# Queries loaded transposed, with maximum and reciprocal sum of each token spread through DRAM

## The chip, the core and the metric

The kernel runs on one NeuronCore of a Trainium2 chip. Its engines are TensorE (matmuls and transposes, called PE in the profile), VectorE (DVE), ScalarE (ACT), GpSimd (POOL) and SyncE (SP), which here only issues DMA transfers. The metric is the device time of one execution in microseconds.

## The reference

Three layers in a row. With B = 8 batches, H = 8 heads, S = 576 tokens and D = 64 features per head:

```python
q_s = exp(q - max(q, axis=-1));  q_s = q_s / (sum(q_s, axis=-1) + 1e-9)   # over the features
k_s = exp(k - max(k, axis=2));   k_s = k_s / (sum(k_s, axis=2) + 1e-9)    # over the tokens
kv = einsum('bhsd,bhse->bhde', k_s, v)
x  = einsum('bhsd,bhde->bhse', q_s, kv)        # attention output, 4608 x 512 when put together
x  = (relu(x @ w_in) ** 2) @ w_out             # 512 -> 2048 -> 512
x  = rms_norm(x) * rms_g
out = (silu(x @ w_gate) * (x @ w_val)) @ w_out2   # 512 -> 1536 -> 512
```

The softmax of q is over the 64 features of one token, so each token of each head has one maximum and one sum. All is float32.

## The kernel before, in words

**Stages.** The attention of batch 0 runs alone. The first product (x @ w_in) of batch b then runs on TensorE, and the attention of batch b+1 is done between its instructions. When all eight batches are through, `down` (@ w_out), the gated products and the last product follow; the change does not touch these.

**The first product.** A batch's product is cut into PA = 8 groups; a group makes two blocks of 128 outputs for all 576 tokens by a scheme with seven block products instead of eight (names B11, T2, T1, B21, T4, B22, T3). Each block product, `product_a`, is two times three matmuls of 128x128 by 128x288 (lines 1814 to 1816: each number is split in a high and a low part), and is one *step*. A batch has 56 steps. In a group the order is B11, T2, T1, B21, then T4 and B22 of the group before, then T3. After each step TensorE does the attention *rounds* that a table puts there. In batch 0's product, where batch 1's attention is done, all eight products are plain ones (64 steps, `plain`, lines 1835 to 1837).

**The attention in units.** A unit (b, c) is a pair of heads, 128 features; there are KC = 4 per batch, so 28 units beside batch 0. For a unit:
- SyncE loads q (tokens on partitions, 5 tokens and two heads a partition), k with features on partitions (kT), k with tokens on partitions (kt) and v.
- DVE takes the maximum of each token (`qmax`, line 1378), POOL subtracts it (`qsub`, 894), ScalarE takes the exponential (`qexp`, 1082), DVE sums and inverts (`qsum`, `qinv`, 1381 to 1388), POOL multiplies (`qnorm`, 897).
- Round Q0 is three and Q1 two transposes on TensorE (line 1803); ScalarE copies them from the bank to qT (1098). Features are then on partitions.
- Round KM transposes the maxima of k (1791), DVE adds them to kt (1415), ScalarE takes the exponential (1079), round KV multiplies with v and a column of ones (1788, ten instructions), DVE divides and writes a 128x128 block-diagonal matrix bd (1402 to 1410).
- Rounds X0 and X1 multiply bd with the halves of qT (1807); ScalarE copies them to xa (1102), the input of the next batch's product. POOL forms sums of xa (`xa_sums`), ScalarE and DVE split it in high and low parts (`ta_split`).

**What sets the order.** The order on each engine is written out. `UNIT_BASE` gives the step of the previous batch's product that is a unit's zero, and the tables `UNIT_PE`, `UNIT_DVE`, ... give each task's distance from it. Engines wait for one another by semaphores, and each works strictly in its order. DVE also takes the first product's results from the banks: in a group of seven steps `h_u2` comes at place 1, `h_21` (waits for product T4) at place 4, `h_12` (waits for B22) at 5, `h_22` (waits for T3) at 6, each ahead of that step's attention tasks. SyncE has one list for everything, and after each group the two stores of h (`store_h`).

**Banks.** Rounds use two banks of the accumulator in turn (`psR`), so a round waits until the result of the round two before it has been read (`wait_bank`). `taken_by_act` tells who reads which round.

The functions that the diff touches:

Of the kernel before, what the change touches and what calls it, by code (L numbers as in the profile page):

```python
# [12 lines left out]
P = 128  # L13
# [160 lines left out]
def taken_by_act(what):  # L174
    return what not in ("KM", "KV")


def taken_no(n):

    act = taken_by_act(ROUNDS[n][1])  # L180
    return act, sum(taken_by_act(what) == act for _, what, _ in ROUNDS[:n + 1])
# [115 lines left out]
def build(nc, q4_d, q1_d, kT_d, k5_d, v4_d, v1_d, w1_d, s1_d, w2_d, wB_d, gv_d, out):  # L297
    h_d = nc.dram_tensor("h_scratch", [P, CA, B * S], F32, kind="Internal").ap()
    xn_d = nc.dram_tensor("xn_scratch", [P, KC, B * S], F32, kind="Internal").ap()
    a_d = nc.dram_tensor("a_scratch", [P, CB, B * S], F32, kind="Internal").ap()  # L300
    ctx = ExitStack()
    with ctx:
# [81 lines left out]
        vn[1], at = place("vn1", at, [P, SJ, P + 1])  # L384
        assert at <= quad_at
# [5 lines left out]
        qT, at = place("qT", at, [P, S])  # L391
# [4 lines left out]
        qmax, at = place("qmax", at, [P, SJ, 2])  # L396
# [39 lines left out]
        q_sum, q_den, q_inv, q_norm = sem("q_sum"), sem("q_den"), sem("q_inv"), sem("q_norm")  # L436
        rnd_ready, taken_act, taken_dve = sem("rnd_ready"), sem("taken_act"), sem("taken_dve")
# [39 lines left out]
        CONSTS, CONSTS_ALONE, CONSTS_Q = 13, 6, 2  # L477
# [10 lines left out]
        def unit(b, c):  # L488
            return b * KC + c + 1

        def bufs(b, c):

            if b == 0:
                return Bufs(kT_al[:, c], qn_al[:, c], vn_al[:, c], ekS_al[:, c], qT_al[:, c], bd_al[:, c],
                            kmax_al[:, c], qmax_al[:, c])
            i = c % 2
            return Bufs(kT[i][:, :], qn[i][:, :, :, :], vn[i][:, :, :], kt[i][:, :, :], qT[:, :], bd[:, :], kmax[:, :],
                        qmax[:, :, :])

        def loads(b, c):  # L500

            if b == 0:
                return (kT_al_in[c], 16), (q_al_in[c], 32), (v_al_in[c], 32)
            n = (b - 1) * (KC // 2) + c // 2 + 1
            return (kT_in[c % 2], 16 * n), (q_in[c % 2], 32 * n), (v_in[c % 2], 32 * n)

# [113 lines left out]
        def _(sp):  # L620
# [11 lines left out]
            def load_q(b, c):  # L632

                if unit(b, c) > KC + 2:
                    sp.wait_ge(rnd_ready, ROUND_NO[b - (c < 2), "Q1", (c - 2) % KC])
                q = bufs(b, c).q.rearrange("p j h d -> p j (h d)")
                sp.dma_start(q[:, 0:FULL], q4_d[b, c]).then_inc(loads(b, c)[1][0], 16)
                sp.dma_start(q[0:TAIL, FULL], q1_d[b, c]).then_inc(loads(b, c)[1][0], 16)
# [152 lines left out]
            def task(what, b, c):  # L791

                if what in ("q", "kT", "kt", "v"):
                    if unit(b, c) > KC + 2:
                        {"q": load_q, "kT": load_k, "kt": load_kt, "v": load_v}[what](b, c)
                elif what == "s1":
# [67 lines left out]
        def _(pool):  # L864
            done = 0
            for fill in (
# [7 lines left out]
                lambda: nc.gpsimd.memset(qn[0][TAIL:P, FULL], 0.0),  # L874
                lambda: nc.gpsimd.memset(qn[1][TAIL:P, FULL], 0.0),
# [12 lines left out]
            def attention(what, b, c):  # L888
# [180 lines left out]
        def _(act):  # L1069
            def attention(what, b, c):  # L1070
                u = unit(b, c)
                m = bufs(b, c)
                if what == "kexp":
# [10 lines left out]
            def take_round(kind, b, c):  # L1084
# [14 lines left out]
                else:  # L1099
                    if b:  # L1100
                        act.wait_ge(ta_lo, split_a(b - 1, B22))
# [45 lines left out]
            def task(what, b, i):  # L1147

                if what[:4] == "read":
                    if what[4:] not in ("KM", "KV"):  # L1150
                        take_round(what[4:], b, i)
# [212 lines left out]
        def _(dve):  # L1364
            def attention(what, b, c):
# [8 lines left out]
                elif what == "qmax":  # L1374
# [3 lines left out]
                    nc.vector.tensor_reduce(m.qmax, m.q, axis=AX.X, op=ALU.max).then_inc(q_max, 1)  # L1378
# [3 lines left out]
                elif what == "qinv":  # L1382
# [3 lines left out]
                    if u > 1:  # L1386
                        dve.wait_ge(q_norm, u - 1)
                    nc.vector.reciprocal(qinv[:, :, :], qden[:, :, :]).then_inc(q_inv, 1)
# [5 lines left out]
            def take_round(kind, b, c):  # L1394
# [6 lines left out]
                if kind == "KV":  # L1401
# [9 lines left out]
                    last.then_inc(taken_dve, 1)  # L1411
                else:
# [356 lines left out]
        def _(pe):  # L1769
            def do_round(kind, b, c):  # L1770
# [320 lines left out]
```

## Time and profile before

| | us |
|---|---|
| median of 3 runs | 1673.07 (1672.58 to 1673.17) |
| the profiled execution, its own time | 1674.19 |
| its span, first to last instruction | 1672.5 |
| attention of batch 0, alone | to about 31 |
| first product with the attention of batches 1 to 7 | about 31 to 420, some 56 a batch |
| busy in the span: PE / DVE / ACT / POOL | 1651.7 / 1156.5 / 617.1 / 595.0 |

Matmuls are pipelined, so their durations overlap in the records; what one costs the stream is read from start times. Idle time of an engine is given in square brackets in a timeline, with what ended it.

### The profile page before, as it was taken

What the parts mean: (1) busy time and instruction counts of PE and PEld (TensorE: products, weight loads), DVE (VectorE), ACT (ScalarE), POOL (GpSimd) and SP (SyncE); (2) the same over time, 40 slices, a digit from 0 to 9 for tenths busy, and PEclk for the clock granted to TensorE, in tenths of its full rate; (3) what the DMA queues carried; (4) which work ended last, traced back from release to release, by engine and by line L of the source; (5) the groups of instructions that cost most, each with busy time, mean ns of one, the idle gap of its engine ahead of it and who ended that gap; (6) DMA issues with size and microseconds to landing.
All of it is one profiled execution on the core that took longest, in us unless ns stands there. A gap on an engine that the chain in (4) does not pass through costs nothing.

```text
span 1672.5 us, 26402 instructions
## 1 busy us (share of the span) xinstructions
PE 1651.7 (99%) x9926; PEld 1510.2 (90%) x9926; DVE 1156.5 (69%) x1749; ACT 617.1 (37%) x1056; POOL 595.0 (36%) x470
## 2 busy tenths in 40 slices
PE   7999999999999999999999999999999998999999
PEld 6999999999988888888888988988998988999999
DVE  6687667666576778888766565556555568877775
ACT  5544334433333323333334333323333344344432
POOL 3554323332102225342247644556455553000000
PEclk9999999999999999999999999999999999999999
DMA  7685546554553454434342323232331344434441
GB/s 251 195 255 174 173 153 193 173 170 146 201 177 88 121 170 126 119 115 127 113 155 72 104 92 111 91 127 82 107 101 57 104 136 163 140 126 151 150 137 56
DMA packets 151743, 230.07 MB, mean 138 GB/s; under 512 B 11840, under 2 KB 75840, under 8 KB 151616
## 3 DMA queue, kind: packets, MB, share of 16 engines
q1 hardware_dynamic: 151616, 228.38, 42.0%
q8 instruction: 80, 1.31, 0.3%
q14 instruction: 47, 0.39, 0.1%
HBM read 143.39 MB, written 84.93 MB: 137 GB/s over the span
## 4 chain that ended last, share of the span: by engine, by line
PE 92%; DVE 2%; POOL 2%; issue 1%; DMA 1%; ACT 1%; SPq 0%; DVEq 0%; POOLq 0%; ACTq 0%
PE bank L1814 16%; PE bank L1815 16%; PE bank L1816 16%; PE bank L1900 7%; PE bank L1901 7%; PE bank L1902 7%; PE bank L1990 5%; PE bank L1992 5%; PE bank L1991 5%; PE bank L1788 2%; PE bank L1807 2%; PE bank L1803 1%; PE bank L1836 1%; PE bank L1835 1%; PE bank L1837 1%
## 5 line engine op out<-in xcount | busy, mean ns | idle before, releaser
L1814 PE MATMUL bank<-TR,SW 128*128 128x512 f32 (+1 forms) x840 | 308.6, 367 | 0.3 <-DVE TR L1553 0.3
L1816 PE MATMUL bank<-TR,SW 128*128 128x512 f32 (+1 forms) x840 | 308.7, 368 | 0.0
L1815 PE MATMUL bank<-TR,SW 128*128 128x512 f32 (+1 forms) x840 | 308.6, 367 | 0.0
L1814 PE MATMUL bank<-TAR,SA 128*128 128x288 f32 x784 | 248.5, 317 | 0.1
L1815 PE MATMUL bank<-TAR,SA 128*128 128x288 f32 x784 | 231.1, 295 | 0.0
L1816 PE MATMUL bank<-TAR,SA 128*128 128x288 f32 x784 | 230.6, 294 | 0.0
L1900 PE MATMUL bank<-GH,W 128*128 128x512 f32 x576 | 224.2, 389 | 0.4 <-DVE GH L1458 0.4
L1901 PE MATMUL bank<-GH,W 128*128 128x512 f32 x576 | 224.2, 389 | 0.0
L1902 PE MATMUL bank<-GH,W 128*128 128x512 f32 x576 | 224.2, 389 | 0.0
L1145 ACT ACTIVATE GH<-g 128x512 fp32r<-128x512 f32 x144 | 91.1, 633 | 241.6 <-DVE g L1453 159.1
L1990 PE MATMUL bank<-SW,OA 128*128 128x256 f32 x630 | 178.9, 284 | 0.2 <-DVE SW L1627 0.2
L1991 PE MATMUL bank<-SW,OA 128*128 128x256 f32 x630 | 178.8, 284 | 0.0
L1992 PE MATMUL bank<-SW,OA 128*128 128x256 f32 x630 | 178.8, 284 | 0.0
L1814 PEld LDWEIGHTS bank<-TR,SW 128*128 128x128 f32 x840 | 157.7, 188 | 20.6 <-DVE TR L1553 0.6
L1815 PEld LDWEIGHTS bank<-TR,SW 128*128 128x128 f32 x840 | 157.7, 188 | 19.9
L1816 PEld LDWEIGHTS bank<-TR,SW 128*128 128x128 f32 x840 | 157.7, 188 | 19.8
L1458 DVE TENSOR_TENSOR GH<-g,GH 128x512 fp32r<-128x512 f32 x144 | 138.6, 963 | 37.9 <-ACT GH L1145 37.8
L1814 PEld LDWEIGHTS bank<-TAR,SA 128*128 128x128 f32 x784 | 147.2, 188 | 3.4 <-issue 0.4
L1815 PEld LDWEIGHTS bank<-TAR,SA 128*128 128x128 f32 x784 | 147.7, 188 | 2.2
L1816 PEld LDWEIGHTS bank<-TAR,SA 128*128 128x128 f32 x784 | 147.3, 188 | 0.0
L1025 POOL TENSOR_TENSOR group<-group,group 128x512 f32<-128x512 f32 (+1 forms) x60 | 73.1, 1219 | 189.8 <-DVE group L1601 189.4
L1900 PEld LDWEIGHTS bank<-GH,W 128*128 128x128 f32 x576 | 108.1, 188 | 23.3 <-DVE GH L1458 0.8
(176 smaller groups left out, 3340.4 us busy)
## 6 DMA issues: line engine op xcount, KB each, us to landing
h_scratch<-hb SPq DMA_DIRECT2D x128, 288.0 KB, 2.6
hst<-h_scratch SPq DMA_DIRECT2D x144, 256.0 KB, 2.7
araw<-a_scratch SPq DMA_DIRECT2D x18, 1536.0 KB, 6.8
a_scratch<-group SPq DMA_DIRECT2D x72, 256.0 KB, 2.0
xst<-xn_scratch SPq DMA_DIRECT2D x10, 1024.0 KB, 5.4
xn_scratch<-x SPq DMA_DIRECT2D x9, 1024.0 KB, 5.4
a_scratch<-group SPq DMA_DIRECT2D x48, 192.0 KB, 1.9
out<-ost SPq DMA_DIRECT2D x36, 256.0 KB, 2.0
```

The costliest lines, as they stand in the source:

```text
L1025: nc.gpsimd.tensor_tensor(a1, a1, val1, ALU.mult).then_inc(a1_done, 1)
L1145: nc.scalar.activation(GH[:, r % GH_RING, 0], g[:, r % G_RING], ACT.Copy).then_inc(ghi_done, 1)
L1458: nc.vector.tensor_tensor(GH[:, r % GH_RING, 1], g[:, r % G_RING], f(GH[:, r % GH_RING, 0]), ALU.subtract)\
L1814: nc.tensor.matmul(ps[:, 0:w], w_hi[:, cc], x_hi[:, c], start=opens and c == 0, stop=False, skip_group_check=True)
L1815: nc.tensor.matmul(ps[:, 0:w], w_lo[:, cc], x_hi[:, c], start=False, stop=False, skip_group_check=True)
L1816: last = nc.tensor.matmul(ps[:, 0:w], w_hi[:, cc], x_lo[:, c], start=False, stop=c == 1, skip_group_check=True)
L1900: nc.tensor.matmul(acc[c][:, :], W2[:, j, 0, cc], GH[:, r % GH_RING, 0], start=j == 0, stop=False, skip_group_check=True)
L1901: nc.tensor.matmul(acc[c][:, :], W2[:, j, 1, cc], GH[:, r % GH_RING, 0], start=False, stop=False, skip_group_check=True)
L1902: last = nc.tensor.matmul(acc[c][:, :], W2[:, j, 0, cc], GH[:, r % GH_RING, 1], start=False, stop=j == CA - 1, skip_group_check=True)
L1990: nc.tensor.matmul(ps, a_hi, w_hi, start=start, stop=False, skip_group_check=True)
L1991: nc.tensor.matmul(ps, a_lo, w_hi, start=False, stop=False, skip_group_check=True)
L1992: last = nc.tensor.matmul(ps, a_hi, w_lo, start=False, stop=stop, skip_group_check=True)
```

## The change

For the units of batches 1 to 7:
- The queries are loaded a second time with features on partitions (`load_qT`, one transfer of 128x576). The load with tokens on partitions is laid out anew: partition p holds tokens 5p to 5p+4 of both heads (115 partitions, and the last token on a 116th); it serves only for maximum and sum.
- `qmax` and `qinv` are written side by side into qs (two buffers). SyncE stores them in DRAM (`store_qs`, 116 partitions of 4 rows of 5 numbers) and loads them back with one row repeated on the 64 partitions of a head: `load_max` into qmax_all and `load_inv` into qinv_all, two transfers each. Both buffers are single, so load_max waits for the unit before's `qTsub` and load_inv for the read of its X1.
- POOL subtracts the maxima from qT (`qTsub`), ScalarE takes the exponential (`qTexp`). POOL's `qnorm`, rounds Q0 and Q1 and ScalarE's copies of them are gone.
- DVE, not ScalarE, reads X0 and X1, and multiplies by the reciprocal sums in doing so.
- Places in the tables: the unit bases become 13, 23, 33, 44 for batch 1 (were 10, 22, 33, 44) and 11, 18, 28, 39 for the others (were 8, 17, 28, 39); the loads and the work on q with tokens on partitions are earlier by 3, relative to the base.

```diff
-UNIT_BASE = [[10, 22, 33, 44]] + [[8, 17, 28, 39]] * (B - 2)
-UNIT_PE = [("KM", -3), ("Q0", 0), ("Q1", 1), ("KV", 2), ("X0", 6), ("X1", 7)]
-UNIT_DVE = [("qmax", -10), ("qsum", -6), ("qinv", -6), ("kmax", -9), ("readKM", -2), ("readKV", 3)]
-UNIT_ACT = [("qexp", -7), ("kexp", -1), ("readQ0", 1), ("readQ1", 2), ("readX0", 7), ("readX1", 8)]
-UNIT_POOL = [("qsub", -9), ("qnorm", -4)]
-UNIT_SP = [("q", -20), ("kT", -19), ("kt", -17), ("v", -15)]
+SHARE = S // SJ
+UNIT_BASE = [[13, 23, 33, 44]] + [[11, 18, 28, 39]] * (B - 2)
+UNIT_PE = [("KM", -3), ("KV", 2), ("X0", 6), ("X1", 7)]
+UNIT_DVE = [("qmax", -13), ("qsum", -9), ("qinv", -9), ("kmax", -9), ("readKM", -2), ("readKV", 3), ("readX0", 7), ("readX1", 8)]
+UNIT_ACT = [("qexp", -10), ("kexp", -1), ("qTexp", 3)]
+UNIT_POOL = [("qsub", -12), ("qTsub", 1)]
+UNIT_SP = [("q", -23), ("kT", -19), ("kt", -17), ("v", -15), ("qT", -9), ("store_qs", -7), ("load_max", -3), ("load_inv", 2)]
...
-def taken_by_act(what):
-    return what not in ("KM", "KV")
+def taken_by_act(b, what):
+    return what not in (("KM", "KV", "X0", "X1") if b else ("KV",))
...
+                    if later(b, c) > 2:
+                        sp.wait_ge(q_sum, unit(b, c) - 2)
+                    else:
+                        sp.wait_ge(const_done, CONSTS_Q1)
+                    q = bufs(b, c).q.rearrange("p j h d -> p (j h) d")
+                    sp.dma_start(q[0:SHARE], q5_d[b - 1, c]).then_inc(loads(b, c)[1][0], 16)
+                    sp.dma_start(q[SHARE:SHARE + 1, 0:2 * SJ:SJ], qe_d[b - 1, c]).then_inc(loads(b, c)[1][0], 16)
+            def load_qT(b, c):
+                if later(b, c) > 2:
+                    sp.wait_ge(rnd_ready, ROUND_NO[b - (c < 2), "X1", (c - 2) % KC])
+                sp.dma_start(bufs(b, c).qT, qT_d[b - 1, c]).then_inc(qT_in[c % 2], 16)
+            def store_qs(b, c):
+                sp.wait_ge(q_inv, unit(b, c))
+                rows = qs_d[unit(b, c) - 1].rearrange("k (p j) -> p k j", j=SJ)
+                sp.dma_start(rows[0:SHARE + 1], qs[0:SHARE + 1, c % 2, :, :]).then_inc(qs_st[c % 2], 16)
+            def spread(b, c, to, first, done):
+                for h in range(2):
+                    row = qs_d[unit(b, c) - 1, first + h:first + h + 1, 0:S]
+                    sp.dma_start(to[h * D:(h + 1) * D, :], row.to_broadcast([D, S])).then_inc(done, 16)
+            def load_max(b, c):
+                sp.wait_ge(qs_st[c % 2], 16 * ((later(b, c) + 1) // 2))
+                if later(b, c) > 1:
+                    sp.wait_ge(qT_sub, later(b, c) - 1)
+                spread(b, c, qmax_all, 0, max_in)
+            def load_inv(b, c):
+                if later(b, c) > 1:
+                    sp.wait_ge(taken_dve, taken_no(ROUND_NO[b - (c < 1), "X1", (c - 1) % KC] - 1)[1])
+                spread(b, c, qinv_all, 2, inv_in)
...
+                elif what == "qTsub":
+                    pool.wait_ge(qT_in[c % 2], 16 * ((b - 1) * (KC // 2) + c // 2 + 1))
+                    pool.wait_ge(max_in, 32 * later(b, c))
+                    nc.gpsimd.tensor_tensor(bufs(b, c).qT, bufs(b, c).qT, qmax_all[:, :], ALU.subtract).then_inc(qT_sub, 1)
...
+                elif what == "qTexp":
+                    act.wait_ge(qT_sub, later(b, c))
+                    nc.scalar.activation(m.qT, m.qT, ACT.Exp).then_inc(qT_exp, 1)
...
+                elif kind in ("X0", "X1"):
+                    cols = slice(int(kind[1]) * TA, (int(kind[1]) + 1) * TA)
+                    dve.wait_ge(ta_lo, split_a(b - 1, B22))
+                    dve.wait_ge(inv_in, 32 * later(b, c))
+                    nc.vector.tensor_tensor(xa[:, c, cols], ps[:, 0:TA], qinv_all[:, cols], ALU.mult).then_inc(taken_dve, 1)
...
                     wait_taken(pe, ROUND_NO[b, "KV", c] - 1)
-                    wait_taken(pe, ROUND_NO[b, "Q1" if half else "Q0", c] - 1)
+                    if b:
+                        pe.wait_ge(qT_exp, later(b, c))
+                    else:
+                        wait_taken(pe, ROUND_NO[b, "Q1" if half else "Q0", c] - 1)
                     last = nc.tensor.matmul(ps[:, 0:TA], m.bd, m.qT[:, half * TA:(half + 1) * TA], start=True, stop=True)
```

`later(b, c)` counts the units from batch 1 on, from 1. The order of the rounds in a batch's 56 steps becomes: 8 KM0; 13 KV0; 15 KM1; 17 X0 of u0; 18 X1 of u0; 20 KV1; 24 X0 of u1; 25 X1 of u1, KM2; 30 KV2; 34, 35 X of u2; 36 KM3; 41 KV3; 45, 46 X of u3.

## Rows read from the trace of the kernel before

**Rows 1.** The page, part 1: busy us (share), instructions.
```profile
PE 1651.7 (99%) x9926; PEld 1510.2 (90%) x9926; DVE 1156.5 (69%) x1749; ACT 617.1 (37%) x1056; POOL 595.0 (36%) x470
```
**Rows 2.** Windows: stretch: length, busy by engine (instructions), PEclk, DMA share, GB/s.
```profile
32.00:40.00 8.00, 7.16 (x55) 6.96 (x54) 5.54 (x10) 4.00 (x8) 2.52 (x2) 1.00 0.89 298
...
208.00:264.00 56.00, 56.00 (x419) 54.90 (x419) 38.74 (x89) 21.52 (x48) 18.98 (x13) 1.00 0.52 170
```
**Rows 3.** The chain of waits in order of time: start, us, what.
```profile
211.56 0.33 PE bank L1803 x3
213.69 1.34 PE bank L1788 x10
...
223.82 1.12 PE bank L1788 x10
...
267.40 0.33 PE bank L1803 x3
```
**Rows 4.** Timeline of TensorE around a unit: start, us, instruction.
```profile
221.12 0.29 PE L1814 MATMUL bank<-TAR,SA 128*128 128x288 f32 x1
...
221.52 0.49 PE L1803 MATMUL bank<-ident,qn 128*128 128x128 f32 x3
...
222.24 0.30 PE L1814 MATMUL bank<-TAR,SA 128*128 128x288 f32 x1
...
222.64 0.38 PE L1803 MATMUL bank<-ident,qn 128*128 128x128 f32 x2
...
223.26 0.30 PE L1814 MATMUL bank<-TAR,SA 128*128 128x288 f32 x1
...
230.12 0.29 PE L1814 MATMUL bank<-TAR,SA 128*128 128x288 f32 x1
...
231.02 0.30 PE L1814 MATMUL bank<-TAR,SA 128*128 128x288 f32 x1
```
**Rows 5.** Line 1803: durations min/median/max; and the timeline at its first later round.
```profile
L1803 PE MATMUL bank<-ident,qn x140: 270/271/329, 39.9 to 413.3; 128*128 128x128 f32 x140
...
38.81 0.29 PE L1837 MATMUL bank<-TAR,SA 128*128 128x288 f32 x1
39.95 0.52 PE L1803 MATMUL bank<-ident,qn 128*128 128x128 f32 x3 [0.84 <-POOL qn L897]
```
**Rows 6.** Groups by line and form, 0 to 560 us: busy us, mean ns, idle before.
```profile
L1504 DVE TENSOR_TENSOR hb<-hb,bank 128x288 f32<-128x288 f32 x56 | 25.4, 454 | 1.9
...
L914 POOL TENSOR_TENSOR xa<-xa 128x576 f32<-128x576 f32 x7 | 10.1, 1436 | 0.0
...
L1128 ACT ACTIVATE TAR<-xa 128x576 fp32r<-128x576 f32 x46 | 30.3, 676 | 12.9 <-POOL xa L920 12.9
```
**Rows 7.** Timelines of TensorE and DVE: end of T4, h_21; then an X round.
```profile
202.33 0.29 PE L1816 MATMUL bank<-TAR,SA 128*128 128x288 f32 x1
...
202.66 0.46 DVE L1491 TENSOR_TENSOR hb<-hb,bank 128x288 f32<-128x288 f32 x1 [0.61 <-PE bank L1816]
203.03 0.93 DVE L1438 TENSOR_TENSOR TAR<-xa,TAR 128x576 fp32r<-128x576 f32 x1
...
227.57 0.29 PE L1814 MATMUL bank<-TAR,SA 128*128 128x288 f32 x1
...
228.85 0.29 PE L1814 MATMUL bank<-TAR,SA 128*128 128x288 f32 x1
```
**Rows 8.** Timelines of SyncE's queue and DVE where the first unit's store would go.
```profile
31.86 2.85 SPq L652 DMA_DIRECT2D SA<-in_w  x5
...
38.24 0.22 DVE L1388 RECIPROCAL qinv<-qden 128x10 f32<-128x10 f32 x1
```
**Rows 9.** DMA issues: count, KB each, median us from issue to landing.
```profile
h_scratch<-hb SPq DMA_DIRECT2D x128, 288.0 KB, 2.6
...
kT<-in_kT SPq DMA_DIRECT2D x28, 288.0 KB, 3.7
...
gv<-in_gv SPq DMA_DIRECT2D x1, 2.0 KB, 6.2
```

More of the change, by code:

```diff
@@ L171 @@
 N_ALONE = len(ALONE_PE) - 1
-def taken_by_act(what):
-    return what not in ("KM", "KV")
+def taken_by_act(b, what):
+    return what not in (("KM", "KV", "X0", "X1") if b else ("KV",))
 def taken_no(n):
-    act = taken_by_act(ROUNDS[n][1])
-    return act, sum(taken_by_act(what) == act for _, what, _ in ROUNDS[:n + 1])
+    act = taken_by_act(*ROUNDS[n][:2])
+    return act, sum(taken_by_act(b, what) == act for b, what, _ in ROUNDS[:n + 1])
 NR = NT * CA
@@ L384, in build @@
         vn[1], at = place("vn1", at, [P, SJ, P + 1])
+        qT = [None] * 2
+        for i in range(2):
+            qT[i], at = place(f"qT{i}", at, [P, S])
         assert at <= quad_at
@@ L390, in build @@
             kt[i], at = place(f"kt{i}", at, [P, SJ, P])
-        qT, at = place("qT", at, [P, S])
+        qmax_all, at = place("qmax_all", at, [P, S])
+        qinv_all, at = place("qinv_all", at, [P, S])
         bd, at = place("bd", at, [P, P])
@@ L505, in loads, with later @@
             return (kT_in[c % 2], 16 * n), (q_in[c % 2], 32 * n), (v_in[c % 2], 32 * n)
+        def later(b, c):
+            return unit(b, c) - KC
         def round_bank(n):
@@ L632, in load_q @@
             def load_q(b, c):
[L634 to L638, printed above, removed]
+                if b == 0:
+                    q = bufs(b, c).q.rearrange("p j h d -> p j (h d)")
+                    sp.dma_start(q[:, 0:FULL], q4_d[c]).then_inc(loads(b, c)[1][0], 16)
+                    sp.dma_start(q[0:TAIL, FULL], q1_d[c]).then_inc(loads(b, c)[1][0], 16)
+                else:
[6 more added lines that the diff above has]
+                    sp.dma_start(q[SHARE:SHARE + 1, 0:2 * SJ:SJ], qe_d[b - 1, c]).then_inc(loads(b, c)[1][0], 16)
@@ L795, in task @@
                         {"q": load_q, "kT": load_k, "kt": load_kt, "v": load_v}[what](b, c)
+                elif what == "qT":
+                    load_qT(b, c)
+                elif what == "store_qs":
+                    store_qs(b, c)
+                elif what == "load_max":
+                    load_max(b, c)
+                elif what == "load_inv":
+                    load_inv(b, c)
                 elif what == "s1":
@@ L1149, in task @@
                 if what[:4] == "read":
-                    if what[4:] not in ("KM", "KV"):
+                    if taken_by_act(b, what[4:]):
                         take_round(what[4:], b, i)
@@ L1377, in attention @@
                         dve.wait_ge(q_sub, u - 1)
-                    nc.vector.tensor_reduce(m.qmax, m.q, axis=AX.X, op=ALU.max).then_inc(q_max, 1)
+                    if b and later(b, c) > 2:
+                        dve.wait_ge(qs_st[c % 2], 16 * ((later(b, c) - 1) // 2))
+                    nc.vector.tensor_reduce(m.qmax.rearrange("p j h -> p (j h)"), m.q.rearrange("p j h d -> p (j h) d"),
+                                            axis=AX.X, op=ALU.max).then_inc(q_max, 1)
                 elif what == "qsum":
@@ L1385, in attention @@
                     dve.wait_ge(q_den, u)
-                    if u > 1:
-                        dve.wait_ge(q_norm, u - 1)
-                    nc.vector.reciprocal(qinv[:, :, :], qden[:, :, :]).then_inc(q_inv, 1)
+                    if b == 0:
+                        if u > 1:
+                            dve.wait_ge(q_norm, u - 1)
+                        nc.vector.reciprocal(qinv[:, :, :], qden[:, :, :]).then_inc(q_inv, 1)
+                    else:
+                        if later(b, c) > 2:
+                            dve.wait_ge(qs_st[c % 2], 16 * ((later(b, c) - 1) // 2))
+                        nc.vector.reciprocal(qs[:, c % 2, 2:4, :].rearrange("p k j -> p (k j)"),
+                                             qden[:, :, :].rearrange("p j h -> p (j h)")).then_inc(q_inv, 1)
                 else:
@@ L2069 @@
     k1 = np.concatenate([k1, k4[:, :, TAIL:, FULL - 1]], axis=2)
+    heads = q.reshape(B, KC, 2, S, D)[1:]
     arrays = {
-        "q4": q4,
-        "q1": q1,
+        "q4": q4[0],
+        "q1": q1[0],
+        "q5": np.ascontiguousarray(heads[:, :, :, 0:SHARE * SJ].reshape(B - 1, KC, 2, SHARE, SJ, D).transpose(0, 1, 3, 2, 4, 5))
+        .reshape(B - 1, KC, SHARE, 2 * SJ, D),
+        "qe": np.ascontiguousarray(heads[:, :, :, SHARE * SJ:].transpose(0, 1, 3, 2, 4)),
+        "qT": np.ascontiguousarray(heads.transpose(0, 1, 2, 4, 3)).reshape(B - 1, KC, P, S),
         "kT": np.ascontiguousarray(k.reshape(B, KC, 2, S, D).transpose(0, 1, 2, 4, 3)).reshape(B, KC, P, S),
```

20 lines of the change are left out of this document (11 added, 9 removed).

## The prediction

> **What bounds the kernel now.** I began with the page's busy shares: TensorE is busy 99% of the span [rows 1]. That row counts overlapping matmuls, so I went on to the stretch table: in 56 us of the attention-and-first-layer stage TensorE has no idle time, DVE is busy 38.7 us, POOL 19.0, and the DMA engines half the time; the granted clock is full, 2.4 GHz [rows 2]. The chain of waits settles it: it runs through TensorE's own instructions, batch after batch, and the same transposes come back after 267.40 - 211.56 = 55.84 us [rows 3]. So each batch's period is the sum of what TensorE streams; an instruction taken from it shortens the period unless a wait comes in its place. Third I read TensorE's timeline by start times, since durations overlap there [rows 4].
>
> **Notation.** One step is one product_a (six matmuls). A batch has 56 steps. u0 to u3 are the four attention units (pairs of heads) of the next batch, worked in between. E13 is the moment at which TensorE has streamed the product of step 13.
>
> **Part 1: five transposes less per unit.** Q0 and Q1 go. Half a product, three matmuls, takes 0.40 us (221.12 to 221.52). Q0 begins at 221.52, and the next product's second half at 222.24: 222.24 - 221.52 - 0.40 = 0.32 us for three transposes and the slower matmul behind them. Q1: 223.26 - 222.64 - 0.40 = 0.22 us [rows 4]. That is 0.54 us a unit, 28 units: -15.1 us. One wait goes too: in the first unit of a batch the KV round takes 1.34 us on the chain instead of 1.12 [rows 3]; its bank is that of Q0, which ScalarE has to read first, and now the round two before it is long read. -0.22 x 6 batches = -1.3. And TensorE's 0.84 us wait for POOL's normalization in the first unit of all goes [rows 5].
>
> A row and a page differ here. The profile gives each transpose a duration of 271 ns [rows 5], but five of them move the stream by 0.54 us only. The Trainium skill, "TensorE: Matmul & The Clock Gate", Part 4, gives about 275 ns for a 128x128 transpose in a kernel's context. By that the 140 transposes would be worth some 38 us; it is a rival below.
>
> **Part 2: X is read by DVE, with the factor.** A DVE operation on a bank of 128x288 takes 454 ns [rows 6], so eight reads add 3.6 us of DVE to 38.7 in a period of 54: no bound. ScalarE loses its copies and gets one exp of 128x576, about 676 ns; POOL's normalization becomes a subtraction of 128x576, 1436 ns [rows 6], about what it was. None of these is on the chain.
>
> But the order of DVE's work is written out, and a bank is now given back later. The banks of the rounds are two, so a round waits for the read of the round two before it. In the new order step 24 ends with X0 of u1, step 25 with X1 of u1 and, right behind it, KM of u2 (28 - 3). KM of u2 takes the bank of X0 of u1. DVE reads that at its step 25, which is the fifth of a group of seven, where h_21 comes first, and h_21 waits for the T4 product that TensorE does in this same step 25. From rows: take s as the start of T4's last matmul (202.33). DVE starts h_21 at s+0.33 and its next operation 0.37 later (203.03), so the read of X0 would run s+0.70 to s+1.15. TensorE streams T4 to s+0.13, X1 costs 227.57 to 228.85 less two halves of products, 1.28 - 0.80 = 0.48, so it is at KM at s+0.61 [rows 7]. It waits 0.54 us, and refilling its pipe costs about one weight load more: I take 0.7 us, once in each of 6 batches: +4.2. Bounds: 0 if the read slips in front of h_21, 1.2 if KM's weights and the next product refill in full. In the batch done beside the plain stage the same pair (step 30) has DVE waiting for the product of step 29, not 30, and fits. KM of u3 comes two steps after X0 of u2, which is enough (2.1 us against 1.6).
>
> **Part 3: the way through DRAM.** Per unit SyncE issues six more transfers: qT, one store of 116 x 20 numbers, four spreading loads. At 0.57 us each [rows 8] that is 14 us more in a period of 54, which alone delays nothing. The cost is in when they land. The trace has no load of one DRAM row into 64 partitions; the nearest, kT with the same 2304 bytes a partition, lands in 3.7 us, a store of h in 2.6, and the smallest, gv (16 bytes a partition) in 6.2 [rows 9]. So 2.6 to 6.2; I take 3.7 for a pair, counted from the second issue.
>
> The tightest unit is u1, whose base lies only 7 steps behind u0's. SyncE has k's load for u2 (step 11) in its queue, and that waits for the KV round of u0, which moved from step 10 to 13. So SyncE stands until E13+1.3 (KV costs 1.12 [rows 3], and its last matmul's tail). Behind it are that load (0.5), load_inv of u0 (1.1), v of u2 in two parts (1.2), two h stores (0.8), and load_max of u1, whose second issue starts at E13+5.5 and lands at E13+9.2. POOL's subtraction and the exp [rows 6] bring it to E13+11.4. TensorE reaches X0 of u1 after 11 steps and KV, KM, X0, X1, KV, with KM's cost 231.02 - 230.12 - 0.80 = 0.10 [rows 4]: 8.8 + 1.12 + 0.10 + 0.96 + 1.12 = 12.1. Slack 0.7 us. load_inv of u0 (second issue E13+2.3) lands at E13+6.0; DVE reads it at E13+6.3, and TensorE would feel that only 1 us later. load_inv of u1 waits for DVE's read of X1 of u0 and lands about 1.5 us before its use. Nobody is late, but with little to spare; the other units have 4 us or more. SyncE's h stores go out some 4 us later, with two groups of buffers behind them. I take 0 for all this, with an upper bound of (6.2 - 3.7 - 0.7) = 1.8 us a batch, 10.8 in all.
>
> The first unit has no slack. Its reciprocal is ready at 38.46 as before, but five weight loads issued from 31.86 on [rows 8] (2.62 MB, at 298 GB/s and 89% of the DMA engines [rows 2] until about 41), and qT, are ahead of its store, so this lands at about 43. load_max's second issue at 43.6 plus 2.6 to 3.7 gives 46.8; subtraction and exp until 48.9. TensorE ends step 10's product at 38.94 (38.81 plus 0.13, [rows 5]) and is at X0, after step 19, at 38.94 + 0.10 + 4.0 + 1.12 + 3.2 = 47.4. Wait about 1.4 us (0 to 4). SyncE is held meanwhile, and s1's load and sums come later: 0.4 more.
>
> **Sum.** Batches 2 to 7: 6 x (-2.16 - 0.22 + 0.70) = -10.1. Batch 1: -2.16 - 0.84 + 1.4 + 0.4 = -1.2. Together -11.3 us. The profiled execution took 1674.19 us (span 1672.5), 1.1 more than the median of 1673.07; 1674.19 - 11.3 - 1.1 = 1661.8 us. What follows the stage is the same work, earlier.
>
> **Rivals.**
> - No new bank wait: DVE's read fits before TensorE gets to KM. For: DVE idles half the time. Against: h_21 is ahead of it in a fixed order. 1661.8 - 4.2, and with a milder start, 1657.
> - Some waits of the spread data: 3.7 us is a median, and the DMA share of 52% [rows 2] comes in bursts. 0.7 to 1.2 us a batch more: 1666 to 1669.
> - Slower than before: the round trip through DRAM is the wait that takes the transposes' place, at X0 of u1 in every batch. It decides once a spreading pair needs over 3.7 + 0.7 = 4.4 us; beyond that each microsecond is one on the chain in each of 6 batches, and before's time is met at 6.3. With 7.5 us it gives 1661.8 + 6 x 3.1 = 1680. For: 64 reads of one row, 464 pieces of 20 bytes, and gv's 6.2 us. Against: kT and h, thirty times the store's bytes and twice a spreading load's, land in 3.7 and 2.6.
> - DVE becomes the bound where it is fullest, beside the plain stage and at batch ends, and eats the gain: about 1672. Against it: it has 17 us idle per period, and kmax leaves the dense end of the batch (step 55 becomes 2 of the next).
> - Transposes are worth their durations: 28 x 5 x 0.271 = 38 us, 1636. The start times speak against it.
>
> The Trainium skill, "DMA: Bandwidth & Descriptors", "Why a DMA increments its semaphore by 16 and not by 1", says that a transfer runs on the largest number of engines up to 16 that divides its outermost dimensions; 116 rows would then use 4 engines, and q's 115 rows 5. All transfers of before have multiples of 16, so no row here shows it. It would put the load of q and the store on few engines; it speaks for the slower rival, though q has ten steps to land.
>
> **Chances.** Forecast 0.56 (its own range 1658 to 1666); no new wait 0.16; some waits 0.13; slower 0.10; DVE 0.04; durations 0.01. 80% range: 1656 (nothing in the transposes' place: 15.1 + 1.3 + 0.8 = 17.2) to 1671. A measurement of this kernel tells 0.2%, 3.3 us, from no change. Faster by more: 0.56 + 0.16 + 0.01 + 0.07 of the waits = 0.80; within: 0.09; slower: 0.11.
>
> **What would show it.** Period of a batch from transposed maxima to the same: 54.1 to 54.3 us instead of 55.84. TensorE idle before KM (the transpose of kmax) about 0.5 to 0.7 us once a batch, released by DVE's read of a bank; none before X0, save once near 47 us, released by ScalarE's exp of qT. SyncE's queue: spreading loads landing in 3 to 4.5 us. Wrong if X rounds wait for the exp in each batch, if DVE waits long for the spread reciprocals, or if the period shrinks by under 1 us.

## The result, and the profile after

Median 1765.95 us of 4 runs (1761.81 to 1775.03), beside 1672.97 for the kernel before: ratio 1.0563, 95% interval 1.0544 to 1.0581. The change costs 93 us; 1661.8 was predicted. The profiled execution took 1768.66 us, span 1766.9.

The page, parts 1 and 4 [rows 1]. TensorE has 140 instructions less and DVE is no busier in share, but the chain that ended last now runs for 10% of the span through transfers (1% before), most of it the store of qs and the spread of the reciprocals:

```profile
PE 1675.7 (95%) x9786; PEld 1523.8 (86%) x9786; DVE 1186.2 (67%) x1805; ACT 593.8 (34%) x972; POOL 598.6 (34%) x470
...
PE 75%; DMA 10%; DVE 6%; POOL 3%; SPq 2%; issue 2%; ACT 1%; DVEq 0%; POOLq 0%; ACTq 0%
PE bank L1893 12%; PE bank L1895 12%; PE bank L1894 12%; PE bank L1979 7%; PE bank L1980 7%; PE bank L1981 7%; PE bank L2069 5%; PE bank L2070 5%; PE bank L2071 5%; DMA qs_scratch<-qs 4%; DMA qinv_all<-qs_scratch 3%; DVE TAR L1514 2%; DMA qmax_all<-qs_scratch 1%; PE bank L1864 1%; PE bank L1886 1%
```

Windows, columns as in [rows 2]. The stretch 208 to 264 has no idle TensorE before; now it loses 6.6 us. At 48 to 64 TensorE stands, and with it so idle the granted clock falls to 0.63 and 0.52 of 2.4 GHz; in the second stretch it is nearly all the time at the lower level, 1.2 GHz:

```profile
48.00:56.00 8.00, 3.70 (x10) 2.61 (x10) 0.00 (x0) 1.39 (x3) 1.40 (x1) 0.63 0.78 254
56.00:64.00 8.00, 4.90 (x22) 4.90 (x23) 4.12 (x7) 3.10 (x4) 4.07 (x5) 0.52 0.74 144
208.00:264.00 56.00, 49.41 (x350) 47.37 (x350) 39.62 (x87) 15.53 (x30) 16.42 (x11) 0.98 0.75 210
```

The period of a batch, read from the starts of the first unit's transposed maxima (line 1867), is 78.2 us for the first and then 64.6 to 74.4; before it is 59.8 and then 55.8 to 56.8. The first product ends at 572.5 us instead of 476.8, so all of the loss lies ahead of that. From 27 us to there, TensorE is idle for 74.4 us (1.7 before), and the granted clock is at 1.2 GHz for 78.5 us, in 16 falls, with TensorE busy in 66.1 of them (never before). At that level ten matmuls of a KV round take 2.16 us instead of 1.12, so I estimate this at half of 66.1, 33 us. Idle time and clock are thus 106 us more, and the stage is 96 us longer: what is left, 10 us, is gained.

DMA issues, median us to landing [rows 9]. Not only are the new transfers slower than the 3.7 I took; the old ones are too (h was 2.6, kT 3.7):

```profile
h_scratch<-hb SPq DMA_DIRECT2D x128, 288.0 KB, 5.0
...
kT<-in_kT SPq DMA_DIRECT2D x28, 288.0 KB, 6.1
...
qmax_all<-qs_scratch SPq DMA_DIRECT2D x56, 144.0 KB, 4.1
qinv_all<-qs_scratch SPq DMA_DIRECT2D x56, 144.0 KB, 5.0
```

Waits between 40 and 420 us (who waited for whom: us, times, longest). The round trip ends at TensorE in two places: at the X round (line 1886) by way of the exp, and, since DVE's read of X (1487) waits for the spread reciprocals, at the next rounds that need its bank, KV (1864) and the transpose of kmax (1867). The product (1893) waits for DVE's split. PE and PEld rows of one line show one wait twice; one of them is shown:

```profile
POOL qT L955 <- DMA qmax_all<-qs_scratch: 139.4, 21, 9.6
...
DVE xa L1487 <- DMA qinv_all<-qs_scratch: 33.3, 10, 10.8
...
PE bank L1886 <- ACT qT L1143: 21.4, 11, 4.7
PEld bank L1893 <- DVE TAR L1514: 21.1, 11, 6.8
...
PEld bank L1867 <- DVE xa L1487: 13.5, 6, 4.3
...
PEld bank L1864 <- DVE xa L1487: 11.8, 5, 2.9
```

The chain in the first unit, and then in a later batch: the store of 9 KB takes 7.55 us to land, the spread of the reciprocals 7.44. SyncE stands for the store, and everything behind it is late. It is no start-up effect: counted from the semaphore events of the trace, the 28 stores land in 3.8 to 10.3 us, 7.5 in the median:

```profile
37.55 7.55 DMA qs_scratch<-qs
45.12 0.46 SPq L674
...
51.03 7.44 DMA qinv_all<-qs_scratch
58.59 0.47 DVE xa L1487
...
197.74 2.16 PE bank L1864 x10
...
200.79 6.92 DMA qinv_all<-qs_scratch
...
212.01 8.72 DMA qs_scratch<-qs
...
225.12 6.94 DMA qs_scratch<-qs
```

And one row that I took long to read rightly, from the timeline of SyncE's queue (start, length of the issue). The issue right behind the store of qs (line 668) takes 6.59 us, where issues take about 0.5:

```profile
143.72 0.34 SPq L668 DMA_DIRECT2D qs_scratch<-qs  x1
144.12 6.59 SPq L641 DMA_DIRECT2D kt<-in_k  x1
150.75 0.59 SPq L694 DMA_DIRECT2D vn<-in_v  x1
```

### The profile page after: what moved, and what is told of

Read it like the earlier page. It is cut to its first block, busy times and chain, and to the rows that moved or that the text cites. A ratio compares the mean times of both kernels' runs of the same rounds, so it can differ in the third digit from the quotient of the medians.

```text
span 1766.9 us, 26259 instructions
## 1 busy us (share of the span) xinstructions
PE 1675.7 (95%) x9786; PEld 1523.8 (86%) x9786; DVE 1186.2 (67%) x1805; ACT 593.8 (34%) x972; POOL 598.6 (34%) x470
## 3 DMA queue, kind: packets, MB, share of 16 engines
q8 instruction: 78, 1.28, 0.3%
## 4 chain that ended last, share of the span: by engine, by line
PE 75%; DMA 10%; DVE 6%; POOL 3%; SPq 2%; issue 2%; ACT 1%; DVEq 0%; POOLq 0%; ACTq 0%
PE bank L1893 12%; PE bank L1895 12%; PE bank L1894 12%; PE bank L1979 7%; PE bank L1980 7%; PE bank L1981 7%; PE bank L2069 5%; PE bank L2070 5%; PE bank L2071 5%; DMA qs_scratch<-qs 4%; DMA qinv_all<-qs_scratch 3%; DVE TAR L1514 2%; DMA qmax_all<-qs_scratch 1%; PE bank L1864 1%; PE bank L1886 1%
## 5 line engine op out<-in xcount | busy, mean ns | idle before, releaser
L1893 PE MATMUL bank<-TAR,SA 128*128 128x288 f32 x784 | 254.1, 324 | 21.9 <-DVE TAR L1514 16.8
L1894 PE MATMUL bank<-TAR,SA 128*128 128x288 f32 x784 | 237.8, 303 | 0.0
L1895 PE MATMUL bank<-TAR,SA 128*128 128x288 f32 x784 | 237.1, 302 | 0.0
L1893 PEld LDWEIGHTS bank<-TAR,SA 128*128 128x128 f32 x784 | 154.2, 197 | 27.9 <-DVE TAR L1514 25.0
L1894 PEld LDWEIGHTS bank<-TAR,SA 128*128 128x128 f32 x784 | 154.2, 197 | 2.7
L1895 PEld LDWEIGHTS bank<-TAR,SA 128*128 128x128 f32 x784 | 153.6, 196 | 0.0
```

The lines of the kernel that those rows point to most:

```text
L1893: nc.tensor.matmul(ps[:, 0:w], w_hi[:, cc], x_hi[:, c], start=opens and c == 0, stop=False, skip_group_check=True)
L1894: nc.tensor.matmul(ps[:, 0:w], w_lo[:, cc], x_hi[:, c], start=False, stop=False, skip_group_check=True)
L1895: last = nc.tensor.matmul(ps[:, 0:w], w_hi[:, cc], x_lo[:, c], start=False, stop=c == 1, skip_group_check=True)
```

## Experiments

Each was timed in 3 rounds against the kernel before, which stayed at 1672.6 to 1673.2. Intervals are of the ratio to it.

**Is it the layout on 115 and 116 partitions?** Edits to the changed kernel; x128 is both, b_q115 puts q's layout alone into the kernel before (the tokens then stand in another order, and the output isn't the reference's; the same holds for b_tr, b_trW and b_trn below).

```diff
# q128 (q5 padded with zeros past row 116)
-sp.dma_start(q[0:SHARE], q5_d[b - 1, c]).then_inc(loads(b, c)[1][0], 16)
-sp.dma_start(q[SHARE:SHARE + 1, 0:2 * SJ:SJ], qe_d[b - 1, c]).then_inc(loads(b, c)[1][0], 16)
+sp.dma_start(q, q5_d[b - 1, c]).then_inc(loads(b, c)[1][0], 16)
# s128
-sp.dma_start(rows[0:SHARE + 1], qs[0:SHARE + 1, c % 2, :, :]).then_inc(qs_st[c % 2], 16)
+sp.dma_start(rows, qs[:, c % 2, :, :]).then_inc(qs_st[c % 2], 16)
```

> The changed kernel (1766 us), with the token-major q of later batches as one load of 128 partitions x 2560 bytes (rows past the 116th are zeros) instead of 115 partitions and a small rest. Theory F (few engines: a transfer whose partition count is no multiple of 16 moves through few DMA engines and holds up everything queued behind it there): most of the 93 us goes, 1680 to 1715, transfers land in 3 to 5 us instead of 5 to 7. Theory V (volume: 25 MB more are too much for the stage): no change, 1760 to 1772. Theory L (the round trip through DRAM has too little slack whatever the queues do): 1745 to 1766.

> The changed kernel, with only the store of maxima and reciprocals done from 128 partitions instead of 116. Theory F with the blame on the store's 464 small pieces: 1690 to 1730. If the q load is what clogs, the store itself saves at most 1 us a unit: 1745 to 1766. Theories V and L: 1760 to 1770.

> Both of the above together. Theory F: 1662 to 1700, at its best the 1662 that was predicted. Theory V: 1760 or so. Theory L: 1740 to 1765.

> The kernel before, with nothing changed but the q load of later batches: 115 partitions x 2560 bytes and a rest, as in the changed kernel (its tokens are permuted for it, the rest of the computation is left as it was). Theory F: transfers behind the q loads land later (4 to 7 us instead of 2.6 to 3.7), but the loads have slack, so 1673 to 1690. Theories V and L: 1673, landing times unchanged.

Measured: q128 1723.34 us (1.0276 to 1.0311), s128 1729.88 (1.0317 to 1.0352), x128 1712.34 (1.0218 to 1.0248), b_q115 1672.84 (0.999 to 1.0009). So the layout is 53.6 us of the 93. Either half brings most of it (42.6 and 36.1), and q's layout costs nothing in a queue that has room. What is left in x128 is 39 us. Theory F had more in mind: q128 and x128 end above its ranges, s128 just inside; b_q115 separates none of the theories.

**Places in the tables, on x128.** x128_split puts DVE's split of B22 first in its step. x128_sp moves two loads later. x128_all is both, with X0 read a step earlier; x128_allb also moves batch 1's units to 16, 26, 35, 45.

```diff
# x128_split
-table.setdefault(start_of(b) + n - STEPS, []).append((what, b, i))
+tasks = table.setdefault(start_of(b) + n - STEPS, [])
+tasks.insert(0 if table is DVE_AT and i == B22 else len(tasks), (what, b, i))
# x128_sp
-UNIT_SP = [("q", -23), ("kT", -19), ("kt", -17), ("v", -15), ...
+UNIT_SP = [("q", -23), ("kT", -19), ("kt", -12), ("v", -11), ...
```

> The x128 kernel (1712 us), with DVE's B22 split ahead of that step's sum, reciprocal and maximum of u1 and the maxima of k, instead of behind them. Theory O (order: what is left of the loss is tasks on DVE and SyncE standing behind another unit's wait): the wait of TensorE for DVE's TAR (33 us in all in x128) goes for the most part; 12 to 18 us less, 1695 to 1702. Theory D (DMA traffic as such, landings of 4 to 6 us, sets the time): 1708 to 1713, since the waits for spread data take the place.

> The x128 kernel, with kt and v loaded 5 and 4 steps later than now (kt -12, v -11), so that SyncE no longer stands before load_max of u1 until the KV round of u0 is through. Theory O: TensorE's wait at X0 of u1, 2.9 us a batch in the trace, goes, but the wait for the B22 split stays: 1695 to 1706. Theory D: 1708 to 1713, since the spreading loads then land just as late beside others.

> Both orders mended, and DVE's read of X0 one step earlier (readX0 at 6), ahead of h_21, so that KM of u2 finds its bank free. Theory O: 6 batches at about 54.3 to 55 us a period instead of 60.6; what stays is the start of batch 1, some 10 us: 1668 to 1680. Theory D: 1700 to 1712.

> As x128_all, with the units of batch 1 placed 3 steps later (2 the third, 1 the fourth), for the first store that lands late behind the weight loads. Theory O: 3 to 6 us less than x128_all, 1664 to 1675. If the start's delay comes in by SyncE's queue and its late s1 loads and not by the unit's own chain: within 1 us of x128_all.

Measured: 1703.83 (1.017 to 1.020), 1728.26 (1.0321 to 1.0351), 1728.80 (1.031 to 1.0358), 1726.09 (1.0299 to 1.0345). The split gains 8.5 us, less than the 12 to 18 I expected: the 33 us of that expectation add the rows of weight load and matmul, which are one wait, 19.9 us between 30 and 480 us. The later loads lose 16, against my expectation, and x128_all and x128_allb, which contain them, end some 50 us above theirs. A reason stands in the waits of SyncE's queue for the store's landing between 100 and 420 us, x128 first, then x128_sp: it now reaches load_max early and stands there with the other loads behind it. That this is the whole of the 16 us is not shown.

```profile
SPq L673 <- DMA qs_scratch<-qs: 29.0, 12, 4.0
```
```profile
SPq L673 <- DMA qs_scratch<-qs: 59.5, 16, 6.1
```

The chain of x128 (start, us, what) shows three ways in which the rest is lost: the split (1513) behind maxima and sums of u1 (1441, 1445), for which TensorE is idle 2.05 us; the round trip, which X0 (1885) waits for, 0.20 us here and 1.64 in the batch before; and the transpose of kmax (1866) behind DVE's read of X0, 0.43 us. A fourth is not on this chain: at 252.56 the KV round is idle for 1.75 us until DVE has read a bank of X (1486).

```profile
234.13 0.74 DVE qs L1441
234.94 1.27 POOL qn L950
...
237.01 0.83 DVE qden L1445
...
238.82 0.76 DVE TAR L1513
...
248.68 6.22 DMA qmax_all<-qs_scratch
255.04 1.45 POOL qT L954
256.51 0.70 ACT qT L1142
...
257.34 0.72 PE bank L1885 x2
...
259.26 0.46 DVE xa L1486
259.77 0.32 PE bank L1866
```

**More lead for the round trip.** On x128_split: maxima, sums and store four steps earlier, in the first unit 11; load_max 2 to 8 steps earlier. DVE's read of X0 also moves one step earlier, and kt and v are loaded 3 and 2 steps later. d_best also has batch 1's units at 16, 26, 35, 45.

```diff
# d_lead; LEAD holds the places of the first two units of batches 2 to 7
+LEAD = {"q": {0: -34}, "qmax": {0: -24}, "qsub": {0: -23}, "qexp": {0: -21}, "qsum": {0: -20}, "qinv": {0: -20},
+        "store_qs": {0: -18}, "load_max": {0: -11, 1: -5}}
-UNIT_DVE = [("qmax", -13), ("qsum", -9), ("qinv", -9), ...
+UNIT_DVE = [("qmax", -17), ("qsum", -13), ("qinv", -13), ...
+UNIT_SP = [("q", -27), ("kT", -19), ("kt", -14), ("v", -13), ("qT", -9), ("store_qs", -11), ("load_max", -6), ("load_inv", 2)]
```

> x128 (both few-partition transfers mended) with DVE's B22 split first in its step, and the chain of the maxima and sums (qmax, qsub, qexp, qsum, qinv) and the store of qs placed 4 steps earlier, for the first unit of a batch 11; load_max 3 to 8 steps earlier, and load k 3 later, v 2 later. Theory O (order and slack: what is left is the round trip that comes due before its data, and DVE's in-order work behind the maxima): the 31 us between 1703.8 and 1673 go for the most part, 1670 to 1690. Theory V (the added traffic itself fills the queue; lead does not help): it stays at 1700 or above.

> d_lead with batch 1's units at steps 16, 26, 35, 45 instead of 13, 23, 33, 44, so that the first round trip has three steps more. Theory O: batch 1 loses some 10 us at 40 to 64 us in x128; 3 to 8 us below d_lead. Theory V: like d_lead, within 3 us.

Measured: 1695.74 (1.0123 to 1.016) and 1690.88 (1.0089 to 1.015). Together these moves help by 8 us, 13 with batch 1's places (the two intervals overlap). d_lead ends above its 1670 to 1690, d_best 4.9 us below d_lead as expected, and 18 us above the kernel before: slack alone isn't all.

**The traffic without its use.** The kernel before with every transfer of the change, and nobody who uses what they bring. The units keep the places of the kernel before, and the store and load_max come 3 steps later, relative to the unit, than in the change. b_tr doesn't wait for the store and spreads rows of the input; in b_trW SyncE waits, and the rows come from the scratch in DRAM, as in the change. b_tr128 is b_tr with q as before and the store from 128 partitions; b_trn is b_tr without the spreading loads.

```diff
# b_tr: store of constants, spreading loads from the input
+sp.dma_start(qTx[:, :], qT_d[b - 1, c]).then_inc(qTx_in, 16)
+sp.dma_start(rows[0:SHARE + 1], src[0:SHARE + 1]).then_inc(qs_st[c % 2], 16)
+for h in range(2):
+    sp.dma_start(to[h * D:(h + 1) * D, :], row.to_broadcast([D, S])).then_inc(done, 16)
# b_trW, ahead of the loads of the maxima
+sp.wait_ge(qs_st[c % 2], 16 * ((n + 1) // 2))
```

> The kernel before with all transfers of the change added to it, at the change's places relative to the unit: q in 115 and 1 partitions (its tokens are permuted, so the output is not the reference's), qT, a store of 116 x 20 numbers (constants) per unit and four spreading loads. No engine uses what they bring, and SyncE never stands for the store's landing. Theory V (traffic alone): most of the 93 us, 1730 to 1765. Theory D (the wait for the round trip and who stands behind it): 1673 to 1685, landings of the other loads 1 to 2 us longer and hidden, as with the q load alone.

> As b_tr, but SyncE waits for the store's landing before it loads the spread maxima back, as in the change; nothing else waits for these transfers. Theory D in the form that SyncE's standing still holds up the other loads behind it: 1690 to 1730. In the form that only the users of the spread data wait (POOL, then TensorE at X0): within 10 us of b_tr. Theory V: the same as b_tr.

> b_tr with q in its old layout of 128 partitions and the store from 128 partitions; the same volume within 2%, no user, no wait for the store. Theory F (transfers of 115 and 116 partitions clog the queue, SyncE's issues then stand 5 to 8 us, and the h stores behind them come late): no issue over 3 us and 1673 to 1685. Theory V (volume): 1710 or above, with landings as in b_tr (6 to 8 us).

> b_tr without the four spreading loads per unit; q in 115 and 1 partitions, qT and the store of 116 partitions stay. If the layout of q and the store is enough to clog the queue: still 1710 or above, with issues of 5 us. If it needs the spreading loads as well (q's layout alone cost nothing in b_q115): 1673 to 1690.

Measured: b_tr 1731.39 (1.0335 to 1.0366), b_trW 1758.42 (1.0482 to 1.0523), b_tr128 1680.04 (1.003 to 1.0067), b_trn 1683.8 (1.005 to 1.0086). This settles the largest part. Traffic that nobody waits for costs 58 us; SyncE's standing for the store, with the rows from the scratch, 27 more (above all its ranges); and with 128 partitions the same traffic costs 7.4. The volume is nearly free, the layout isn't, and it needs a full queue: without the spreading loads it costs 11.

Timeline of SyncE's queue, b_tr and then b_tr128. The load of v stands for 5.51 us behind the 116-partition store, and not behind the other:

```profile
203.13 0.27 SPq L665 DMA_DIRECT2D qs_scratch<-ident  x1
203.45 5.51 SPq L684 DMA_DIRECT2D vn<-in_v  x1
```
```profile
220.28 0.38 SPq L658 DMA_DIRECT2D qs_scratch<-ident  x1
220.71 0.58 SPq L677 DMA_DIRECT2D vn<-in_v  x1
```

Counted in these timelines between 40 and 470 us, issues directly behind the store against all others: b_tr 21 of 27 over 2 us, mean 4.14, others 0.51; the changed kernel 11 of 24, mean 2.94, others 0.52; q128 10 of 27, mean 1.68; with the store on 128 partitions (s128, x128, b_tr128, d_best) none of 27 each, mean 0.55 to 0.64. The table of waits puts some of this down to TensorE, since v's load also names its semaphore; but the KV round that it needs had ended 3.8 to 13.5 us before the issue began in every one of the long ones, and in the changed kernel, where k's load is the one behind the store, 1.5 to 8.8 us. What suffers is in b_tr's waits: h's buffers come free late, so ScalarE reads the product banks late, and batch 0's sums get their data late.

```profile
ACT hb L1211 <- DMA h_scratch<-hb: 53.1, 12, 8.9
...
POOL SA L967 <- DMA SA<-in_s: 35.2, 7, 8.4
```

Windows of b_tr and of b_tr128: the DMA share is 0.82 and 0.89, they move 208 and 226 GB/s, and TensorE loses 4.1 and 1.4 us. The mended layout moves more in the same time, not less.

```profile
208.00:264.00 56.00, 51.88 (x388) 50.44 (x386) 35.47 (x82) 20.03 (x44) 17.68 (x12) 1.00 0.82 208
```
```profile
208.00:264.00 56.00, 54.58 (x407) 53.24 (x407) 37.07 (x85) 20.62 (x46) 17.44 (x13) 1.00 0.89 226
```

**One spread instead of two.** e_one, on d_best: the logarithm of the sums is added to the maxima, one number per token is spread, X needs no factor.

```diff
+nc.scalar.activation(qden[:, :, :], qden[:, :, :], ACT.Ln).then_inc(q_ln, 1)
+nc.vector.tensor_tensor(qm, qm, qden[:, :, :].rearrange("p j h -> p (j h)"), ALU.add).then_inc(q_inv, 1)
-spread(b, c, qinv_all, 2, inv_in)
```

> d_best with two spreading loads per unit instead of four: ScalarE takes the logarithm of the sums, DVE adds it to the maxima, that sum is stored (2 rows of numbers instead of 4) and spread, and exp(qT - spread) is the normalized query. X needs no factor and is read by ScalarE as in the kernel before. Theory V2 (what is left of the loss in d_best, 18 us, is queue volume and the load on DVE): 1672 to 1683. Theory O (it is the round trip itself, its latency): within 4 us of d_best, 1687 to 1695.

Measured 1692.2 (1.0097 to 1.0129), as d_best. The second spread's waits are gone, but the logarithm has its own price: ScalarE's timeline has 61 table loads of 1.28 us (ACT_TABLE_LOAD), 28 of them ahead of the logarithms and most others ahead of the exponentials that follow, where d_best has 5. The chain has 1.10 us of one on ScalarE just ahead of the logarithm of 0.21 and, behind both, the read of a product bank for which TensorE waits:

```profile
224.31 1.10 ACT L1148
225.61 0.21 ACT qden L1148
225.82 0.31 ACT hb L1242
226.17 0.40 PE bank L1897
```

**Finer places, and a queue of its own.** f_fine, on d_best: u0's maximum and sum 5 steps earlier, u1 one step later with its sum behind the split, reciprocals loaded as soon as the buffer is free. g_act is d_best with store and spreads issued by ScalarE; h_act is g_act with f_fine's places in batches 2 to 7.

```diff
# f_fine
-UNIT_BASE = [[16, 26, 35, 45]] + [[11, 18, 28, 39]] * (B - 2)
+UNIT_BASE = [[16, 26, 35, 45]] + [[11, 19, 28, 39]] * (B - 2)
+        "load_inv": {0: -5, 1: 1, 2: 0, 3: -2}, "readX0": {0: 7}}
# g_act
-sp.dma_start(to[h * D:(h + 1) * D, :], row.to_broadcast([D, S])).then_inc(done, 16)
+nc.scalar.dma_start(to[h * D:(h + 1) * D, :], row.to_broadcast([D, S])).then_inc(done, 16)
```

> d_best, and: maximum and sum of the first unit of a batch 5 steps earlier (out of the splits at the end of the batch before), those of the second unit behind the split of B22, the second unit one step later (its X0 and the next KM then take different banks one step apart), and the loads of the reciprocals issued as soon as the buffer is free (in the first unit 7 steps earlier). Theory O (the rest is DVE's order and the second spread's latency): a batch takes 54 to 55 us instead of 56.1, batch 1 loses 3 us less: 1675 to 1682. Theory V (queue volume): within 4 us of 1690.9.

> d_best with the store of qs and the four spreading loads issued by ScalarE on a queue of its own, at the same steps; SyncE keeps all other transfers. If the shared queue holds the round trip up (it lands in 4 to 5 us behind other loads, and SyncE stands for the store while loads wait behind it): the store and the spreads land in 2.5 to 3.5 us and the time falls to 1670 to 1682. If the DMA engines themselves are the limit: landings stay at 4 to 5 us, 1687 to 1695. Should ScalarE's standing for the store hold up its reads of the product banks: above 1695.

> g_act with f_fine's places for batches 2 to 7 (maximum and sum of the first unit earlier, the second unit one step later, reciprocals loaded as soon as their buffer is free). Shared queue as the cause: 2 to 8 us below g_act, as the wait for the reciprocals of the second unit goes. Engines as the cause: within 3 us of g_act. ScalarE standing: as g_act or worse.

Measured: 1693.2 (1.0107 to 1.0167), 1715.79 (1.0231 to 1.0266), 1727.96 (1.0309 to 1.034). f_fine fails: the waits only change places. g_act answers the question of the queue. On ScalarE's own queue the two spreads together land no sooner than in d_best (4.0 and 4.9), so it isn't SyncE's queue alone that holds them:

```profile
qmax_all<-qs_scratch ACTq DMA_DIRECT2D x56, 144.0 KB, 4.8
qinv_all<-qs_scratch ACTq DMA_DIRECT2D x56, 144.0 KB, 4.2
```

ScalarE's standing for the store comes on top: TensorE's product waits 14.3 us in 12 waits for ScalarE's reads of the banks between 40 and 480 us (5.1 in 7 in d_best). That this is all of the 25 us over d_best is not shown. In h_act the X rounds wait 30.2 us in 6 waits behind DVE's work on kt, a loss of its own. No version beat the kernel before.

## Why the prediction was wrong

**Part 1, the transposes: right.** 0.54 us a unit. Chain of the kernel before, KV of u2 and of u3, then of d_best where nothing waits: 11.50 and 10.96 us for the same 11 steps.

```profile
235.31 1.12 PE bank L1788 x10
246.81 1.12 PE bank L1788 x10
```
```profile
248.58 1.12 PE bank L1868 x10
259.54 1.12 PE bank L1868 x10
```

Over 28 units that is an estimate of 15 us, and in every version it is eaten; the count over the stage of the changed kernel leaves 10. The 271 ns of a transpose in the records, and the Trainium skill's about 275 ("TensorE: Matmul & The Clock Gate", Part 4), are not what one costs the stream.

**Part 2, DVE: place right, bounds too small.** DVE takes 452 ns for an X, as taken. KM waits for DVE's read of X0, forecast at 0.7 us a batch, 4.2 in all: 13.5 us in 6 waits in the changed kernel, since X0 itself is late there; in x128 it is still 10.1 in 8. The KV round, which needs such a bank too, I had not priced: 11.8 us in 5 waits. And I left out DVE's written order: when maxima are late, the split of B22 stands behind them (21.1 us of waits; in x128 16.8, and 8.5 us back with the order changed). "No bound" was argued from DVE's busy share, and that says nothing of an engine that works in order.

**Part 3, the round trip: this step failed.** I wrote "I take 0 for all this", with 1.8 us a batch as upper bound, and of the six more transfers a unit that the time to issue them "alone delays nothing". All three signs that I had named for being wrong came: X rounds wait for the exp, DVE waits for the reciprocals up to 10.8 us, and the period grows. Three terms were wrong.
- The landing of the new transfers was taken from rows of a half-empty queue. DMA share was 0.52 [rows 2]; the traffic of the change takes it to 0.75, and a spread lands in 4.1 to 5.0 where I took 3.7. The maxima's 4.1 would still have fitted the 4.4 us that I named as the turning point, and the reciprocals' 5.0 is about what the 1 to 1.5 us that I gave them allow. The larger miss is the store: past the first unit I gave it no wait at all, and held against the slower rival that kT and h land in 3.7 and 2.6. It lands in 7.5 us in the median (5.1 on 128 partitions, x128), and SyncE stands for it.
- The other transfers were taken as unmoved. They are slower by 2.4 us in the median (h, kT), and SyncE's issues behind the store stand 2.9 us in the mean, so its h stores are late as well. SyncE's slack was large, which is why I counted its issues as free; the stands behind the store use it up. Its longest waits between 40 and 480 us, before and after: before it waited for h's data 199.3 us in all, and now it stands for the store and has 43.1 left of the other.

```profile
SPq L674 <- DVE hb L1497: 199.3, 49, 7.0
```
```profile
SPq L674 <- DMA qs_scratch<-qs: 45.4, 21, 4.2
SPq L723 <- DVE hb L1573: 43.1, 17, 5.3
```

- The layout. I named the Trainium skill's rule ("DMA: Bandwidth & Descriptors", "Why a DMA increments its semaphore by 16 and not by 1"), by which 116 rows use 4 engines and 115 rows 5, and then gave it no term. The profile doesn't say which engine carries a packet, but the semaphore events of the trace do show fewer parts: the landing of a 116-row store comes in 5 updates and that of q's two loads in 9, where every transfer on 64 or 128 partitions has 16. The runs agree with the rule in what 128 partitions change: 53.6 us with the round trip in use, 51.4 without (1731.39 - 1680.04).

**The first unit.** Forecast: store landed at 43, wait 1.4 us. It landed at 45.1 and the spread of the reciprocals, for which I had forecast no wait, at 58.5, behind nine other issues. TensorE stood and its clock fell: between 40 and 96 it was idle for 12 us (busy 44.03 of 56) at a mean granted clock of 0.82, and the first period is 18 us longer than before.

**The rivals.** The slower one named the right mechanism and place, with chance 0.10 and 1680 us. Its price was one wait a batch; the real one includes what the same traffic does to the loads and stores that were there. How the 93 us add up: 58 for traffic that nobody uses (7 of them volume), 27 for SyncE standing for the store, and 8 left for the use of the data less 15 gained. The split is by subtraction of runs with different waits and places, so the last term is not shown by itself, and the order matters: on 128 partitions the traffic alone costs 7 of x128's 39 us, and waits and use the other 32. The estimate in the section on the result cuts the same 93 us another way: a third of it is the clock that falls when TensorE stands. Open is also why the issue behind the 116-partition store stands: that it does is shown, that it waits for room on the few engines is argued. And open are the last 18 us of d_best, for which no run leaves one cause.

## What to carry to other kernels

A transfer added to a busy queue must be priced twice: its own landing in the new load, and what it does to every transfer behind it; adding the traffic alone, with no user, measures the second in one run. Lay even the smallest transfer over 128 partitions: a 9 KB store on 116 held up the next issue by 2.9 us in the mean. And a step moved through DRAM needs its lead from the slowest landing seen (10.3 us for this store), with nothing else queued behind its wait; in an engine with a written order, being late hits whatever stands behind.

## What the runs showed of the hardware

- An issue behind a store of 464 pieces of 20 bytes from 116 partitions takes up to 8.5 us; behind one of 512 pieces from 128, at most 1.7. It also needs a full queue: mean 4.1 us with the spreading loads, 2.1 without them (b_trn).
- Giving the spreads a second queue changed their landing by under 1 us (4.0 and 4.9 to 4.8 and 4.2).
- 64 partitions reading one row of 2304 bytes (144 KB) land in 4.0 and 4.9 us at 0.83 of the engines' time, the 288 KB of kT in 5.7 (d_best).
- Semaphore updates per landing: 5 for a store of 116 partitions, 16 for one of 128 (changed kernel, x128).
- A logarithm among exponentials cost two table loads of 1.28 us each time in e_one: 61 loads in all, against 5 in d_best.
- Where TensorE stood, its granted clock fell to 1.2 GHz, 16 times in the changed kernel's stage (78.5 us in all) and not once before; ten matmuls then took 2.16 us instead of 1.12.
